# Fused attention and two expert layers: one-hot transposes packed, the key mask moved to ScalarE, and a new order of attention

## What is computed

```python
q_assign = np.argmax(np.einsum('bhsd,hcd->bhsc', q_n, c_n), axis=-1)
k_assign = np.argmax(np.einsum('bhsd,hcd->bhsc', k_n, c_n), axis=-1)
mask = q_assign[:, :, :, None] == k_assign[:, :, None, :]
scores = scale * np.matmul(q, k.transpose(0, 1, 3, 2))
scores = np.where(mask, scores, -1000000000.0)
attn = softmax(scores)
out = np.matmul(attn, v)
```

## Time and profile before

| | us |
|---|---|
| runs | 1130.89, 1134.22, 1133.42 |
| median | 1133.42 |
| profiled execution | 1133.1 |
| its span (first to last instruction) | 1131.3 |
| attention, first score product to last write of X | 23.5 to 325.3 |
| TensorE busy over the span | 1071.7 (95%) |
| VectorE busy | 523.4 (46%) |
| ScalarE busy | 417.6 (37%) |
| GpSimd busy | 214.9 (19%) |

### The profile page before, as it was taken

The page is one execution under the profiler, slowest core; times in us unless marked ns, Lnnn a source line. Parts: engine busy times, 40 slices in busy tenths (PEclk is TensorE's granted clock), DMA queues, the critical chain, the costliest instruction groups (busy, mean ns, idle before and its releaser), DMA issues.

```text
span 1131.3 us, 19022 instructions
## 1 busy us (share of the span) xinstructions
PE 1071.7 (95%) x6794; PEld 977.1 (86%) x6794; DVE 523.4 (46%) x1139; ACT 417.6 (37%) x881; POOL 214.9 (19%) x210
## 2 busy tenths in 40 slices
PE   4999999999987799999999999999999999999996
PEld 3888888888876689999899999889999988999995
DVE  2799999999936435554012222222222222222222
ACT  2687778777742224444422221201222120121110
POOL 5132323223110011111413310301111030110022
PEclk9999999999997699999999999999999999999999
DMA  2323131323121714555962120101002000000011
GB/s 72 85 64 99 49 97 51 95 61 85 28 113 46 245 37 166 186 189 175 258 190 75 40 75 1 43 31 37 37 0 74 0 0 0 0 0 0 0 56 56
DMA packets 41352, 82.48 MB, mean 73 GB/s; under 512 B 4704, under 2 KB 10848, under 8 KB 41056
## 3 DMA queue, kind: packets, MB, share of 16 engines
q1 hardware_dynamic: 38608, 75.61, 21.9%
q0 software_dynamic: 2704, 6.33, 1.8%
HBM read 63.02 MB, written 6.32 MB: 61 GB/s over the span
## 4 chain that ended last, share of the span: by engine, by line
PE 79%; ACT 8%; DVE 6%; issue 4%; DMA 1%; POOL 0%; DVEq 0%; ACTq 0%; SPq 0%
PE ps_h L1284 8%; PE ps_h L1286 8%; PE ps_h L1285 8%; PE ps_y L1285 8%; PE ps_y L1286 8%; PE ps_y L1284 8%; PE ps_h L1311 8%; PE ps_y L1326 7%; PE ps_t L1187 2%; ACT probs L593 2%; PE ps_m L1145 2%; PE ps_s L1174 2%; PE ps_o L1201 2%; PE ps_s L1175 2%; ACT p_hi L606 2%
## 5 line engine op out<-in xcount | busy, mean ns | idle before, releaser
L679 ACT ACTIVATE h_hi<-ps_h 128x384 fp32r<-128x384 f32 x128 | 63.0, 492 | 337.2 <-PE ps_h L1286 337.2
L1284 PE MATMUL ps_h<-xs_hi,a_hi 128*128 x512 | 171.3, 335 | 0.0
L1286 PE MATMUL ps_h<-xs_lo,a_hi 128*128 x512 | 171.2, 334 | 0.0
L1285 PE MATMUL ps_h<-xs_hi,a_lo 128*128 x512 | 171.1, 334 | 0.0
L950 DVE SCALAR_TENSOR_TENSOR h_lo<-ps_h,h_hi 128x384 fp32r<-128x384 f32 x128 | 71.4, 558 | 195.6 <-ACT h_hi L679 195.6
L1100 DVE SCALAR_TENSOR_TENSOR X<-ps_y,mix_n,X 128x512 f32 x96 | 72.1, 751 | 189.4 <-PE ps_y L1286 189.4
L1286 PE MATMUL ps_y<-b_lo,h_hi 128*128 128x512 f32 x384 | 149.7, 390 | 0.0
L1285 PE MATMUL ps_y<-b_hi,h_lo 128*128 128x512 f32 x384 | 149.7, 390 | 0.0
L1284 PE MATMUL ps_y<-b_hi,h_hi 128*128 128x512 f32 x384 | 149.4, 389 | 0.0
L868 DVE TENSOR_TENSOR p_lo<-ps_t,p_hi 128x384 fp32r<-128x384 f32 x192 | 102.5, 552 | 14.3 <-ACT p_hi L606 11.0
L606 ACT CAST p_hi<-ps_t 128x384 fp32r<-128x384 f32 x192 | 86.3, 484 | 32.8 <-PE ps_t L1187 32.3
(11 more groups left out here) (175 smaller groups left out, 1700.7 us busy)
## 6 DMA issues: line engine op xcount, KB each, us to landing
raw_a<-in_moe_w_dram SPq DMA_DIRECT2D x16, 1024.0 KB, 5.6
raw_b<-in_moe_w_dram SPq DMA_DIRECT2D x16, 1024.0 KB, 9.3
odd_a<-in_moe_w_dram SPq DMA_DIRECT2D x8, 1024.0 KB, 7.8
odd_b<-in_moe_w_dram SPq DMA_DIRECT2D x8, 1024.0 KB, 12.7
khhT<-kT SPq DMA_DIRECT2D x32, 192.0 KB, 2.9
raw_k<-in_k_dram SPq DMA_DIRECT2D x16, 192.0 KB, 2.6
raw_q<-in_q_dram SPq DMA_DIRECT2D x16, 192.0 KB, 2.6
raw_v<-in_v_dram SPq DMA_DIRECT2D x16, 192.0 KB, 3.2
```

The costliest lines, as they stand in the source:

```text
L1284: t_.matmul(dst, w_hi, x_hi, start=first, stop=False)
L1285: t_.matmul(dst, w_lo, x_hi, start=False, stop=False)
L1286: return t_.matmul(dst, w_hi, x_lo, start=False, stop=last)
```

## The change

- kT and qT become the two halves of one buffer kqT of 12 tiles. `tr_rows` makes three groups of four tiles; the middle one holds two tiles of k and two of q and is copied out in two pieces.
- one_c is laid out so that one transpose takes in four tiles, each with 16 columns at the start of a 32-column block; `tr_own` makes three transposes of 128x128 in place of twelve. The two tiles of k come out on partitions 0 to 15 and 32 to 47, those of q on 64 to 79 and 96 to 111, 384 columns each.
- For keys VectorE writes not-equal in place of equal, in an instruction of its own, and ScalarE makes the key mask by multiplying with -2^100. `copy_own` and `copy_far` are replaced by `copy_own_q` and `copy_far_k`, two copies each.
- `row_scale` runs once per head on all six tiles.
- The lists of steps of TensorE, VectorE and ScalarE are written anew, and on SyncE the loads stand one place earlier.

The diff, cut where lines only follow from these (declarations, counts of semaphores in waits that follow from the new number of groups):

```diff
@@ -340,12 +341,12 @@
 with sp.Fori(0, H - 1) as h:
+    load_head(h + 1, 0)
     key_parts(h, 1)
     query_part(h, 1)
-    load_head(h + 1, 0)
+    load_head(h + 1, 1)
     key_parts(h + 1, 0)
     query_part(h + 1, 0)
-    load_head(h + 1, 1)
@@ -567,18 +568,33 @@
     n, h, b = at
-    act.wait_ge(tr_full, 4 * n + c + 1)
+    act.wait_ge(tr_full, 3 * n + c + 1)
     if c == 0:
         at_least(act, s_full, TPB * (n - 1))
-    dst = (kT, qT)[c // 2][b][:, (c % 2) * HC:(c % 2 + 1) * HC]
-    s.mul(dst, ps_m[:, 0:HC], SCALE if c >= 2 else 1.0).then_inc(tr_copied, 1)
-
-def copy_own(at):
+        s.copy(kqT[b][:, 0:4 * P], ps_m[:]).then_inc(tr_copied, 1)
+    elif c == 1:
+        s.copy(kqT[b][:, 4 * P:6 * P], ps_m[:, 0:2 * P]).then_inc(tr_copied, 1)
+        s.mul(kqT[b][:, 6 * P:8 * P], ps_m[:, 2 * P:4 * P], SCALE).then_inc(tr_copied, 1)
+    else:
+        s.mul(kqT[b][:, 8 * P:12 * P], ps_m[:], SCALE).then_inc(tr_copied, 1)
+
+def copy_own_q(at):
     if not live(at):
         return
     n, h, b = at
-    act.wait_ge(own_full, 2 * n + 1)
-    s.copy(qcT[b][D:D + C, :], ps_m[D:D + C, 0:S // 2].bitcast(BF16)).then_inc(own_copied, 1)
+    act.wait_ge(own_full, n + 1)
+    for i in range(2):
+        src = ps_m[(2 + i) * 32:(2 + i) * 32 + C, 0:HC // 2]
+        s.copy(qcT[b][D:D + C, i * HC:(i + 1) * HC], src.bitcast(BF16)).then_inc(own_copied, 1)
+
+def copy_far_k(at):
+    if not live(at):
+        return
+    n, h, b = at
+    act.wait_ge(own_full, n + 1)
+    for i in range(2):
+        src = ps_m[i * 32:i * 32 + C, 0:HC // 2]
+        s.mul(kcT[b][D:D + C, i * HC:(i + 1) * HC], src.bitcast(BF16), FAR).then_inc(own_copied, 1)
@@ -623,42 +639,42 @@
 def turn(h, b):
-    past, now, soon, later = (near(h, b, d) for d in range(-1, 3))
-    hi_half(now, 1, 1)
-    exp_tile(now, 3)
-    hi_half(now, 2, 1)
-    exp_tile(now, 4)
-    hi_half(now, 3, 0)
-    take_oT(past, 1)
-    copy_own(soon)
-    hi_half(now, 3, 1)
-    hi_half(now, 4, 0)
-    exp_tile(now, 5)
-    hi_half(now, 4, 1)
+    now, soon, later = (near(h, b, d) for d in range(3))
     hi_half(now, 5, 0)
-    take_low(past, 1)
+    exp_tile(soon, 0)
+    copy_tr(later, 0)
+    take_oT(now, 0)
+    hi_half(soon, 0, 0)
     hi_half(now, 5, 1)
-    exp_tile(soon, 0)
-    take_oT(now, 0)
-    copy_tr(later, 0)
+    copy_tr(later, 1)
     exp_tile(soon, 1)
-    copy_tr(later, 1)
-    hi_half(soon, 0, 0)
+    take_low(now, 0)
     hi_half(soon, 0, 1)
-    take_low(now, 0)
     exp_tile(soon, 2)
     hi_half(soon, 1, 0)
     copy_tr(later, 2)
-    copy_tr(later, 3)
+    hi_half(soon, 1, 1)
+    exp_tile(soon, 3)
     hi_half(soon, 2, 0)
+    hi_half(soon, 2, 1)
+    exp_tile(soon, 4)
+    take_oT(now, 1)
+    copy_own_q(later)
+    hi_half(soon, 3, 0)
+    hi_half(soon, 3, 1)
+    copy_far_k(later)
+    hi_half(soon, 4, 0)
+    exp_tile(soon, 5)
+    take_low(now, 1)
+    hi_half(soon, 4, 1)
 for n in range(-2, 2):
     turn(n // 2, n % 2)
 with act.Fori(1, H - 1) as h:
     turn(h, 0)
     turn(h, 1)
-for n in range(NHEAD - 2, NHEAD + 1):
-    turn(n // 2, n % 2)
+turn(H - 1, 0)
+turn(H - 1, 1)
@@ -837,18 +853,13 @@
     link(v_.tensor_reduce(best_c[:], hit2_c[:], AX.X, ALU.max))
-    at_least(dve, own_full, 2 * m)
-    v_.tensor_tensor(one_c[:, :, D:D + C], hit2_c[:], spread(best_c[:], 2, shape),
-                     ALU.is_equal).then_inc(one_ready, 1)
-
-def copy_far(at):
-    if not live(at):
-        return
-    m, h, b = at
-    dve.wait_ge(own_full, 2 * m + 2)
-    at_least(dve, s_full, TPB * (m - 1))
-    v_.tensor_scalar(kcT[b][D:D + C, :], ps_m[D:D + C, 0:S // 2].bitcast(BF16), -1.0, -FAR, ALU.add,
-                     ALU.mult).then_inc(own_copied, 1)
+    at_least(dve, own_full, m)
+    for i, op in ((0, ALU.not_equal), (1, ALU.is_equal)):
+        ts = slice((1 - i) * TPB, (2 - i) * TPB)
+        v_.tensor_tensor(one_c[:, :, 2 * i:2 * i + 2, 0:C].rearrange("p g j c -> p j g c"),
+                         hit2_c[:, ts, :].rearrange("p (j g) c -> p j g c", j=2),
+                         spread(best_c[:, ts], 2, [P, TPB, C]).rearrange("p (j g) c -> p j g c", j=2),
+                         op).then_inc(one_ready, 1)
@@ -868,55 +879,52 @@
-def row_scale(at, u):
+def row_scale(at):
     if not live(at):
         return
     n, h, b = at
-    U = 2 * n + u
-    dve.wait_ge(exp_done, HALF * U + HALF)
-    v_.tensor_scalar(den[:], row_sum[:, 2 * b + u, :], 1e-9, None, ALU.add).then_inc(x_step, 1)
-    dve.wait_ge(x_step, 3 * U + 1)
+    dve.wait_ge(exp_done, TPB * n + TPB)
+    v_.tensor_scalar(den[:], row_sum[:, 2 * b:2 * b + 2, :].rearrange("p u g -> p (u g)"), 1e-9, None,
+                     ALU.add).then_inc(x_step, 1)
+    dve.wait_ge(x_step, 4 * n + 1)
     v_.reciprocal(rden[:], den[:]).then_inc(x_step, 1)
 def rows_out(at, u):
     if not live(at):
         return
     n, h, b = at
-    U = 2 * n + u
-    dve.wait_ge(low_done, U + 1)
+    dve.wait_ge(low_done, 2 * n + u + 1)
     v_.tensor_tensor(o_sum[:], ps_m[:, 0:HC].rearrange("p (j m) -> p j m", m=P)[:, :, 0:D],
                      o_low[:], ALU.add).then_inc(x_step, 1)
-    dve.wait_ge(x_step, 3 * U + 3)
+    dve.wait_ge(x_step, 4 * n + 3 + u)
     t0 = b * TPB + u * HALF
     v_.tensor_tensor(X[:, t0:t0 + HALF, bass.ds(h * D, D)], o_sum[:],
-                     spread(rden[:], 2, [P, HALF, D]), ALU.mult).then_inc(x_done, 1)
+                     spread(rden[:, u * HALF:(u + 1) * HALF], 2, [P, HALF, D]), ALU.mult).then_inc(x_done, 1)
 def turn(h, b):
     now, soon, later = (near(h, b, d) for d in range(3))
-    max_tile(soon, 3)
     max_tile(soon, 4)
-    lo_half(soon, 2, 0)
     lo_half(soon, 1, 1)
     cluster_sums(later)
     own_cluster(later)
+    lo_half(soon, 2, 0)
     lo_half(soon, 2, 1)
+    max_tile(soon, 5)
     lo_half(soon, 3, 0)
-    max_tile(soon, 5)
     lo_half(soon, 3, 1)
     lo_half(soon, 4, 0)
-    copy_far(later)
-    row_scale(now, 1)
+    max_tile(later, 0)
+    rows_out(now, 1)
+    lo_half(soon, 5, 0)
+    row_scale(soon)
     lo_half(soon, 4, 1)
-    max_tile(later, 0)
-    lo_half(soon, 5, 0)
-    rows_out(now, 1)
     max_tile(later, 1)
+    lo_half(later, 0, 0)
     lo_half(soon, 5, 1)
-    row_scale(soon, 0)
     max_tile(later, 2)
-    lo_half(later, 0, 0)
     rows_out(soon, 0)
     lo_half(later, 0, 1)
+    max_tile(later, 3)
@@ -1116,21 +1124,22 @@
     n, h, b = at
-    if c % 2 == 0:
-        pe.wait_ge(rows_split, 3 * n + c // 2 + 1)
     if c == 0:
+        pe.wait_ge(rows_split, 3 * n + 1)
         at_least(pe, x_done, 2 * n - 4)
         if isinstance(n, int):
-            at_least(pe, own_copied, 2 * n)
-    elif c == 2:
-        pe.wait_ge(tr_copied, 4 * n + 2)
+            at_least(pe, own_copied, 4 * n)
+    elif c == 1:
+        pe.wait_ge(rows_split, 3 * n + 2)
+        pe.wait_ge(tr_copied, 4 * n + 1)
+    else:
+        pe.wait_ge(tr_copied, 4 * n + 3)
         at_least(pe, x_done, 2 * n - 3)
-    else:
-        pe.wait_ge(tr_copied, 4 * n + c)
-    src = (k_rows, q_rows)[c // 2][b]
-    for j in range(HALF):
+    for j in range(4):
+        t = 4 * c + j
         mm = t_.transpose(ps_m[:, j * P:(j + 1) * P].bitcast(F32R),
-                          src[:, (c % 2) * HALF + j].rearrange("p a d -> p (a d)"), ident_r[:])
+                          (k_rows, q_rows)[t // TPB][b][:, t % TPB].rearrange("p a d -> p (a d)"),
+                          ident_r[:])
@@ -1146,17 +1155,14 @@
-def tr_own(at, i):
+def tr_own(at):
     if not live(at):
         return
     n = at[0]
-    if i == 0:
-        pe.wait_ge(one_ready, n + 1)
-    else:
-        pe.wait_ge(own_copied, 2 * n + 1)
-    for j in range(TPB):
-        mm = t_.transpose(ps_m[0:D + C, j * D:(j + 1) * D].bitcast(BF16), one_c[:, i * TPB + j, :],
-                          ident_b[:])
+    pe.wait_ge(one_ready, 2 * n + 2)
+    for g in range(HALF):
+        mm = t_.transpose(ps_m[:, g * D:(g + 1) * D].bitcast(BF16),
+                          one_c[:, g].rearrange("p j c -> p (j c)"), ident_b[:])
@@ -1165,7 +1171,7 @@
         pe.wait_ge(parts_in[b], 64 * (h + 1))
-        pe.wait_ge(own_copied, 2 * n + 2)
+        pe.wait_ge(own_copied, 4 * n + 4)
@@ -1222,37 +1228,35 @@
     past, now, soon, later = (near(h, b, d) for d in range(-1, 3))
-    values(past, 1, 0)
-    tr_probs(now, 2, 1)
-    values(past, 1, 1)
-    tr_probs(now, 3, 0)
-    tr_own(soon, 0)
-    scores(now, 5)
-    tr_probs(now, 3, 1)
-    tr_probs(now, 4, 0)
-    tr_own(soon, 1)
-    values(now, 0, 0)
+    tr_out(past, 1)
     tr_probs(now, 4, 1)
     tr_probs(now, 5, 0)
-    scores(soon, 0)
-    tr_out(past, 1)
-    tr_probs(now, 5, 1)
-    scores(soon, 1)
     values(now, 0, 1)
     tr_rows(later, 0)
+    scores(soon, 1)
+    tr_probs(soon, 0, 0)
+    tr_probs(now, 5, 1)
+    tr_rows(later, 1)
     scores(soon, 2)
-    tr_rows(later, 1)
-    tr_probs(soon, 0, 0)
+    tr_out(now, 0)
     tr_probs(soon, 0, 1)
-    tr_out(now, 0)
+    tr_probs(soon, 1, 0)
     scores(soon, 3)
-    tr_probs(soon, 1, 0)
     tr_rows(later, 2)
```

(30 more changed lines are left out.)

## The result

The changed kernel takes 1120.84 us (median of 4 runs, 1119.93 to 1125.16) against 1133.77 (4 runs, 1130.89 to 1134.22): a ratio of 0.9899, 95% interval 0.9868 to 0.9929. It is faster by 12.9 us; 1120.0 was forecast. The profiled execution took 1119.93 us, its span is 1118.1.

The account below looks back on a forecast made before the run. A chain through bank ps_m, with no engine full, was taken to set the 18.36 us period. Gains of 12.0 (periods), 1.2 (front) and 0.3 (drain), 13.5 us, gave 1119.6 profiled, forecast 1120.0; range 1112 to 1130.

Parts of the forecast that it names:

- The sum 16.1 + 1.3: TensorE's period per head: 16.1 us of issued steps plus 1.3 us of waits, 17.4, taken as 17.5.
- The walk: New order stepped from scores(0) to the next head's scores(0), which it put at 17.45 us.
- the signs named: Profile signs: TensorE's X waits about 1 us, one-hots about 4, VectorE 89% busy; mask wait above 1 us a head wrong.
- q copies after the output copy 14.9 to 15.7 ... key copies to 17.4: Walk's last step on ScalarE: q copies, two hi halves to 16.6, key copies, then next scores(0) at 17.45 us.
- The term of the periods: Gain over 14 attention periods: (18.36 - 17.5) x 14 = 12.0 us.
- The mask on ScalarE: Four 16x384 copies at 0.48 us replace one of 0.79: +1.14 us on ScalarE; VectorE loses 0.955.
- Rows by four: ScalarE's row copies: 1.93 us for 1.96, no change of busy time, one ps_m round trip less.
- The front: From first one-hot transposes to first scores: 2.5 us for 3.7, so 1.2 us less.
- The drain: The 17.0 us after X of head 14, to attention's end, loses some hand-overs: 0.3 us.
- A: Rival: TensorE still waits 2.0 us a period at the same links; period 18.1, 1128.6 us; chance 0.17.
- C: Rival, slower: late cluster sums or ScalarE copies at the one-hots lengthen the period; 1137.1 us at x = 1.3; chance 0.10.
- B: Rival, all packs: TensorE waits only 0.6 us, period 16.7, 1108.7 us; chance 0.08.

Follow-up runs that it names:

- the fastest kernel: Changed kernel with the key mask on VectorE and lists turned so scores 0 and output transposes go ahead of probs (4,0), among other swaps: 1105.83 us, ratio 0.9765.

## Why the prediction was right, and where it was not

*What bounds.* The reading that not an engine's load but a chain sets the period held: 13 us less of VectorE's work in 250 changed nothing while the rows went by three, and one copy costs its whole length or nothing by its place. That the chain goes through ps_m is shown for two of its links, the fourth row copy (0.56 us a head) and the stretch of ScalarE behind the q copies. In the fastest kernel TensorE waits most for exponentials, and not for ps_m.

*The sum 16.1 + 1.3.* The steps as priced add up to 16.2, not 16.1, and the 1.13 us of the earlier trace rows are six value products alone, without transposes; they were used as such. In the walk's own steps, the period from 182.32 to 200.10 us has waits of 0.35 us ahead of the output transposes, 0.2 ahead of the second probs group, 0.5 ahead of probs (4,0), 0.65 ahead of scores 0 and 0.1 at the other places: 1.8 us (an estimate: start of a step less the start and the price of the one before), and steps of 16.0. The same estimate gives 2.1 and 16.3 for the kernel before (one-hots at 186.44 to one-hots at 204.88). So the steps were priced right, and the waits came down by 0.3 us a head and not by 0.7. By the measure of the earlier trace rows, which counts weight loads that wait while products still run, they went up from 2.0 to 2.5. The walk had no wait at all for the lo half at probs (4,0), 0.2 for the mask where 0.65 came, and 0.3 for the one-hots where none came.

*The walk.* Set against the trace of one period, from scores 0 at 182.32 to scores 0 at 200.10, and the next one for the first steps, in us from scores 0:

| step of TensorE | walk | trace |
|---|---|---|
| first rows | 2.8 | 2.91 |
| second rows | 4.6 | 4.64 |
| output transposes, first half | 6.1 | 6.14 |
| third rows | 8.2 | 8.13 |
| clusters | 9.8 | 9.53 |
| one-hot transposes | 14.2 | 13.73 |
| probs (4,0) | 16.95 | 16.89 |
| scores 0 of the next head | 17.45 | 17.78 |

The hand-worked order is right to 0.1 us over the first half, and 0.5 us ahead at the one-hots (without the waits of 0.1 at scores 4 and 0.3 at the one-hots). The gain up to there was then lost between the one-hots and scores 0. Of the signs named, the waits for X are 4.3 us and not about 1, those at the one-hots 2.3 and not about 4, VectorE is 86% busy and not 89%; the wait at the mask, 7.7 us or 0.6 a head, stayed below the 1 us that would have been wrong.

*The step that failed* is "q copies after the output copy 14.9 to 15.7 ... key copies to 17.4". I let two 16x384 copies take 0.8 us, start to start 0.4, the lower end of what the walk gave a hi half; from the start of one pair to the instruction behind it they take 0.99 and 1.01 (197.00 to 197.99, 198.88 to 199.89 above). And scores 0 follow the last copy by 0.23 us (199.87 to 200.10), where the walk had the general hand-over of 0.05. That is 0.6 us more than priced on the path. The half microsecond by which the one-hots were early gave only 0.2 of it back, because the exponential of tile 4 and the output copy stand ahead of the q copies and end at 196.97. The rest is the 0.3 us between 17.45 and 17.78. The term of the periods was 12.0 and measured 8.9.

*The mask on ScalarE* was priced at +1.14 us of ScalarE, and each copy measured 0.472 to 0.480 (the earlier trace rows gave 0.48), so the busy time was right and the overlap wrong. The Trainium skill ("ScalarE: Activation LUTs", What ACT_TABLE_LOAD costs) says that back-to-back activations overlap by about 93 ns. The trace agrees roughly for the two row copies of 256 columns below, where the second starts 0.12 us before the first ends, and not for the pairs of mask and q copies, whose two take 0.97 to 0.99 us at 0.472 to 0.480 each:

```profile
205.51 0.39 ACT L576 CAST kqT<-ps_m 128x256 fp32r<-128x256 f32 x1
205.78 0.41 ACT L577 ACTIVATE kqT<-ps_m 128x256 fp32r<-128x256 f32 x1
```

*The packed one-hots* were taken as 0.2 us and measure 196.20 - 196.05 = 0.15 between the starts of their neighbours. *The split comparison* takes 0.254 us apiece for 0.258 forecast. *The single reciprocal* saves what was said and is worth 0.07 us in time. *Rows by four*: one round trip less stood as a remark without a price in the sum by parts; it is worth 0.56 us a head in the new lists, more than any other part tried here.

*The front* was 1.2 us for the one-hot passage of head 0. Scores 0 of head 0 start at 22.66 instead of 23.51, 0.85 us earlier. Where the other 2.0 us come from is shown in part. At the one-hots of head 1 the lead is 38.60 - 37.33 = 1.27 us, so 0.4 came on the way there and 1.65 behind them. In the kernel before a low clock begins at that place, which I left out: there the granted clock was 0.95 from 30 to 40 us and 0.88 from 40 to 50, and products of 384 columns at 39.3 to 42.2 took 0.53 instead of 0.34 us. That is a stretch at 1.2 GHz whose records in the windows amount to 0.5 + 1.2 = 1.7 us of full speed. It began behind a wait of TensorE for one_c of 1.54 us; the changed kernel waits 1.95 us at the same place and keeps the full clock, so the wait alone does not explain it. From the windows and the timeline of TensorE of the kernel before:

```profile
30.00:40.00 10.00, 8.14 (x54) 7.29 (x53) 7.51 (x15) 7.27 (x16) 0.00 (x0) 0.95 0.54 139
40.00:50.00 10.00, 9.66 (x63) 8.65 (x61) 7.59 (x13) 6.64 (x16) 3.62 (x4) 0.88 0.01 2
```

```profile
38.60 0.53 PE L1158 MATMUL ps_m<-ident_b,one_c 128*80 128x128 bf16 x6 [1.54 <-DVE one_c L841]
...
39.34 0.53 PE L1175 MATMUL ps_s<-khhT,qT 128*128 128x384 f32 x1
```

That the clock gives the 1.65 us is argued and not shown, as no run changes it alone. The kernel with the turned lists and the mask on VectorE (16.78 a head) lacks as much in these windows (0.86 and 0.97), with other lists, and still writes its first X at 47.63. In the changed kernel both windows show 1.00:

```profile
30.00:40.00 10.00, 8.05 (x54) 7.47 (x53) 8.36 (x18) 7.39 (x17) 0.00 (x0) 1.00 0.45 124
40.00:50.00 10.00, 9.53 (x65) 8.25 (x65) 8.16 (x16) 9.52 (x23) 0.00 (x0) 1.00 0.25 61
```

*The drain* gave 0.2 for 0.3 forecast. *The rivals.* A (the waits stay, 18.1) was nearer than I had it: 17.72 lies a third of the way from 17.5 to its 18.1. C, the slower case, did not come, but its mechanism is real: in the old lists the mask copies on ScalarE do make the period longer, by 0.37 us, and held up by an exponential, not by the cluster sums. B's 16.7 a head, thought out of reach, is within 0.1 us of what the turned lists gave.

## What to carry to other kernels

In a stage of three in-order engines that hand one bank around, a part and the order of steps have no price by themselves: rows by four cost 0.2 us a head in one order and won 0.56 in the other. Walk the new order step by step with measured starts, and price what stands in the queue behind each wait; then look at what each waiting engine could have done in that time: the lists turned to fill TensorE's wait took the period from 17.82 to 16.78, more than the whole change, though which of the swaps did it was not taken apart. Before two periods are compared, look for a low clock inside them: two periods of 14 made an order look 0.2 us a head worse than it is. Where two copies follow each other, take their distance from a pair of the same shape, not from another one.

## What was not expected of the hardware

- Two copies of 16x384 from the bank to the same partitions do not overlap: 0.97 and 0.99 us for two of 0.47 to 0.48 on ScalarE, while pairs of 128x384 take 0.86 for two of 0.485 and pairs of 128x256 overlap by 0.12. On VectorE two take 1.13 us for 0.55 each. What makes the difference (16 partitions, bf16 as the source, or the partitions read) was not tried.
- In two of the profiled executions a low clock came inside the 14 periods, with single periods 1.4 to 1.7 us longer (20.11 and 19.83 for 18.4) or 1.1 (19.43 for 18.35), and in none of the others.
- The part behind attention, with the same instructions in all kernels, takes between 801.2 and 808.4 us. This is larger than most of the differences that single runs were to show.
